# Tail of a two-layer FFN on one core: VectorE's h cos(h) goes to SBUF, GpSimd takes the tail's low parts, and 16 unread products are dropped

## What is computed

```python
h = np.maximum(x @ w_in, 0.0);  x = h * h @ w_out        # layer 1
h = x @ w_in2;  g = h * np.cos(h);  return g @ w_out2    # layer 2
```

## Time and profile before

| what | value |
|---|---|
| median of 3 runs | 1177.63 us |
| the profiled execution, its own time | 1177.56 us |
| its span, first to last instruction | 1175.7 us |
| TensorE busy (matmuls) | 1172.7 us, 100% |
| VectorE, ScalarE, GpSimd busy | 960.4, 806.1, 366.3 us |
| granted TensorE clock, mean | 1.000 |
| the tail, first L1254 to last used product | 1127.1 to 1170.75 us |

### The profile page before, as it was taken

The page is one execution under the profiler, slowest core; times in us unless marked ns, Lnnn a source line. Parts: engine busy times, 40 slices in busy tenths (PEclk is TensorE's granted clock), DMA queues, the critical chain, the costliest instruction groups (busy, mean ns, idle before and its releaser), DMA issues.

```text
span 1175.7 us, 25787 instructions
## 1 busy us (share of the span) xinstructions
PE 1172.7 (100%) x9953; PEld 1132.5 (96%) x9954; DVE 960.4 (82%) x1504; ACT 806.1 (69%) x1467; POOL 366.3 (31%) x265
## 2 busy tenths in 40 slices
PE   9999999999999999999999999999999999999999
PEld 7989999999999999999999999999999999999988
DVE  7968899878878787887878878787787878878787
ACT  4977666667667666666766666676666767666676
POOL 4993634070420706125070430705215070000000
DMA  8511111110111101111011111101111000100001
GB/s 214 135 51 30 35 28 35 17 37 15 23 35 28 35 11 19 35 28 35 15 19 34 25 35 28 35 9 21 35 28 35 13 17 3 26 2 15 1 1 28
DMA packets 113174, 37.33 MB, mean 32 GB/s; under 512 B 101662, under 2 KB 110878, under 8 KB 113052
## 3 DMA queue, kind: packets, MB, share of 16 engines
q1 hardware_dynamic: 111100, 34.87, 14.2%
q10 hardware_dynamic: 1952, 0.80, 0.3%
HBM read 23.84 MB, written 6.29 MB: 26 GB/s over the span
## 4 chain that ended last, share of the span: by engine, by line
PE 100%; issue 0%; DVE 0%
PE y L608 51%; PE h L608 46%; PE y L713 1%; PE h L630 1%; PE h L1121 0%; PE h L637 0%; PE y L674 0%; PE h L640 0%; PE h L644 0%; PE h L1123 0%; PE y L675 0%; PE y L676 0%; PE y L725 0%; DVE g_hi L1543 0%; PE y L659 0%
## 5 line engine op out<-in xcount | busy, mean ns | idle before, releaser
L608 PE MATMUL y<-g_hi,wo 64*128 64x512 f32 x3048 | 698.2, 393 | 0.2
L608 PE MATMUL y<-g_lo,wo 64*128 64x512 f32 x2032 | 521.1, 391 | 0.0
L608 PEld LDWEIGHTS y<-g_hi,wo 64*128 64x128 f32 x3048 | 420.5, 184 | 14.5 <-PE y L608 1.1
L529 POOL TENSOR_TENSOR tap<-xc,gen 128x768 f32<-128x768 f32 x98 | 150.9, 1546 | 575.3 <-DVE xd_lo L1522 555.2
L608 PEld LDWEIGHTS y<-g_lo,wo 64*128 64x128 f32 x2032 | 305.3, 184 | 2.0
L1179 ACT ACTIVATE turns<-turns 128x512 f32<-128x512 f32 x238 | 150.2, 631 | 182.4 <-DVE turns L1473 182.4
L608 PE MATMUL h<-xa_hi,wa_hi 64*128 64x512 f32 x1018 | 270.6, 397 | 0.1
L608 PE MATMUL h<-xa_hi,wa_lo 64*128 64x512 f32 x1018 | 266.0, 391 | 0.0
L608 PE MATMUL h<-xa_lo,wa_hi 64*128 64x512 f32 x1018 | 265.5, 391 | 0.0
L1493 DVE TENSOR_TENSOR h<-h,turns 128x512 f32<-128x512 f32 x238 | 165.6, 696 | 114.6 <-ACT turns L1179 114.2
L1467 DVE SCALAR_TENSOR_TENSOR h<-h,relu 128x512 f32<-128x512 f32 x249 | 173.4, 696 | 57.2 <-ACT relu L1154 55.0
(11 more groups left out here) (127 smaller groups left out, 1092.7 us busy)
## 6 DMA issues: line engine op xcount, KB each, us to landing
xc<-in_x_dram SPq DMA_DIRECT2D x60, 240.0 KB
out_dram<-arena SPq DMA_DIRECT2D x62, 64.0 KB, 1.9
xt_a<-x_blocks SPq DMA_DIRECT2D x224, 16.0 KB, 1.8
arena<-in_moe_w_out_dram SPq DMA_DIRECT2D x16, 192.0 KB, 3.7
arena<-in_moe_w_in_dram SPq DMA_DIRECT2D x16, 128.0 KB, 2.5
out_dram<-arena SPq DMA_DIRECT2D x62, 32.0 KB, 1.7
xt_d<-x_blocks SPq DMA_DIRECT2D x112, 16.0 KB, 1.8
arena<-in_moe_w_in_dram SPq DMA_DIRECT2D x16, 64.0 KB, 2.9
```

Of the source, the lines that this page charges most:

```text
L529: pool.tensor_tensor(tap[:, k % 2, :].rearrange("p (r g) -> p r g", g=GROUP), rows[k], wk, ALU.mult).then_inc(pool_step, 1)
L608: return pe.matmul(o, w[rows, :], x[rows, :], start=start, stop=stop)
```

## The change

In the tail, the product writes 2 pi h cos(h) to SBUF, in `tail_g` (the memory of layer 1's `relu`); the high part is a plain copy of that, and the low part is `tail_g` minus `g2_hi`. The low parts of chunks 238 to 253 are made by GpSimd, those of 254 and 255 by VectorE. TensorE's waits for a free bank go over to the product (`g2_made`), save for the first two such chunks, 240 and 241, whose banks are last read outside the tail's code. VectorE's product waits for the low part of two chunks before, which reads the same half of `tail_g`. The 16 unread products are left out.

```diff
+        tail_g = relu
...
+        POOL_LOWS = range(TAIL - LAG, STEPS - 2)
...
+            for m in POOL_LOWS:
+                pool.wait_ge(g2_hi_ready, m + 1)
+                if m == POOL_LOWS[0]:
+                    pool.wait_ge(g2_ready, m)
+                pool.tensor_tensor(g2_lo[:, m % 2, :], tail_g[:, m % 2, :], g2_hi[:, m % 2, :],
+                                   ALU.subtract).then_inc(g2_ready, 1)
...
-                pe.wait_ge(g2_ready, m - 2)
+                pe.wait_ge(g2_made, m - 2)
...
-                        pe.wait_ge(g2_ready, m - 3)
+                        pe.wait_ge(g2_ready if m - 4 < TAIL - LAG else g2_made, m - 3)
...
-            spare = g2_hi[:, 0, :]
-            line = spare[:, 0:4].unsqueeze(1).to_broadcast([P, TOK // 4, 4])
-            pairs = spare.rearrange("p (b n two) -> p n b two", b=2, two=2)
-            lines = spare.rearrange("p (b n four) -> p n b four", b=2, four=4)
-            for j, moving in enumerate((line, pairs, lines)):
-                for _ in range(4):
-                    pe.matmul(h[:, j, :], wo[1][:, j, 0:P], moving, start=True, stop=True)
-            for _ in range(4):
-                pe.matmul(h[:, 3, :], wo[1][:, 3, 0:DD].bitcast(mybir.dt.bfloat16),
-                          spare[:, 0:TOK // 2].bitcast(mybir.dt.bfloat16), start=True, stop=True)
...
-                        act.activation(g2_hi[:, 1 - c, cols], h[:, tail_bank(m - 1 + part), cols], ACT.Copy,
-                                       scale=2.0 * math.pi).then_inc(g2_hi_ready, 1)
+                        act.activation(g2_hi[:, 1 - c, cols], tail_g[:, 1 - c, cols],
+                                       ACT.Copy).then_inc(g2_hi_ready, 1)
...
-                if m > TAIL - LAG:
+                if m > POOL_LOWS[-1] + 1:
+                    dve.wait_ge(g2_ready, m - 1)
                     for part, cols in parts(m - 1):
                         dve.wait_ge(g2_hi_ready, m + part)
-                        dve.scalar_tensor_tensor(g2_lo[:, 1 - c, cols], h[:, tail_bank(m - 1 + part), cols],
-                                                 2.0 * math.pi, g2_hi[:, 1 - c, cols], ALU.mult,
-                                                 ALU.subtract).then_inc(g2_ready, 1)
+                        dve.tensor_tensor(g2_lo[:, 1 - c, cols], tail_g[:, 1 - c, cols], g2_hi[:, 1 - c, cols],
+                                          ALU.subtract).then_inc(g2_ready, 1)
                 if m < STEPS:
+                    if m >= TAIL - LAG + 2:
+                        dve.wait_ge(g2_ready, m - 1)
                     for part, cols in parts(m):
-                        o = h[:, tail_bank(m + part), cols]
                         dve.wait_ge(cos_ready, m + 1 + part)
-                        dve.tensor_tensor(o, o, wave[:, c, cols], ALU.mult).then_inc(g2_made, 1)
+                        dve.scalar_tensor_tensor(tail_g[:, c, cols], h[:, tail_bank(m + part), cols], 2.0 * math.pi,
+                                                 wave[:, c, cols], ALU.mult, ALU.mult).then_inc(g2_made, 1)
```

## The result

The changed kernel takes 1179.55 us (median of 22 runs, 1179.43 to 1179.70), the kernel before in the same comparison 1177.66 us: 1.89 us more, a ratio of 1.0016 with a 95% interval of 1.0010 to 1.0021. The forecast was 1178.8 us: the side was right, and the cost of the change was put at 1.1 us instead of 1.89.

What follows compares the result with a forecast made beforehand. TensorE was taken to bound the kernel, with VectorE off the path. Gains of 0 and four tail stops totalling 1.14 us on 1177.56 gave 1178.70; the median's 0.07 made it 1178.8 us, range 1177.4 to 1180.8.

Steps and rivals of the forecast that it cites:

- TensorE is the bound, and VectorE's time is off the path: Tail: TensorE sets the pace; 11.0 us less on VectorE only becomes idle time, since products wait for sines: gain 0.
- GpSimd's 1.30 us and the way of 2.05 us: Tail: 1.30 us per GpSimd low part; 2.05 us from high part's start to matmul, 0.60+0.08+1.30+0.07.
- Which chunks: Tail: TensorE stops at chunks 238 (0.55 us), 242 (0.29), 244 (0.16) and 252 (0.14), none at the others.
- steady slots: Tail slots for which chunk 250 stands: low part ready at 1159.68 against matmul at 1159.80, so no stop.
- the forecast's own rule: Tail, per chunk: high part's start plus 2.05 us against the start of the matmul reading the low part; the excess stops TensorE.
- The sum: Whole kernel: stops in the tail total 1.14 us, added to 1177.56 us; with the median's 0.07, 1178.8 us.
- Product and high part in SBUF for nothing: Tail: product written to SBUF, no change; high part read from SBUF, at most 0.02 us a chunk, counted as nothing.
- The end products for nothing: Kernel's end: leaving out the 16 unread products gains 0, as the output does not need them; bounds 0 and 0.9 us.
- The rival that GpSimd paces the tail: Tail: longer GpSimd low parts lose time every two slots; 1181.7 us at 1.85 us each, deciding from 1.65; chance 0.14.
- the margin of 0.12 us: Steady tail slots, read from chunk 250: the low part is ready 0.12 us before its matmul; thin, but no stop.

## Why the prediction was right

*TensorE is the bound, and VectorE's time is off the path: right.* VectorE lost 9.6 us of work and nothing came earlier; its products still start behind sines (12.9 us of waits for L1265).

*GpSimd's 1.30 us and the way of 2.05 us: right.* It measured 1297 ns in the mean. For chunk 238 the high part starts at 1130.16 and the matmul at 1132.22: 2.06 us.

*Which chunks.* 238, 242, 244 and 252 were forecast and are there, in the order of size forecast, and steady slots such as that of 250 have no stop. 248 was not forecast. The run with ScalarE's code moved shows that it is the late issue of its high part: put on time, the stop goes. ScalarE of the kernel before already had that high part 0.66 us behind its L1254, where chunk 249 has 0.51 (its rows, and TensorE's matmul that reads the low part of 248):

```profile
1152.42 0.60 ACT L1254 ACTIVATE turns<-h 128x512 int32<-128x512 f32 x1 [0.44 <-PE h L608]
1153.08 0.60 ACT L1261 ACTIVATE g_hi<-h 128x512 fp32r<-128x512 f32 x1
...
1154.73 0.60 ACT L1254 ACTIVATE turns<-h 128x512 int32<-128x512 f32 x1 [0.32 <-PE h L608]
1155.24 0.60 ACT L1261 ACTIVATE g_hi<-h 128x512 fp32r<-128x512 f32 x1
...
1155.06 0.39 PE L608 MATMUL y<-g_lo,wo 64*128 64x512 f32 x1
```

By the forecast's own rule, 1153.08+2.05 = 1155.13 against 1155.06 is a stop of 0.07. I had read one steady chunk for all. The other 0.17 of its 0.24 us come from the high part, which is later still in the changed kernel (0.84 instead of 0.66).

*The sum: short by 0.75 us.* Forecast were stops of 0.55, 0.29, 0.16 and 0.14; the slots grew by 0.67, 0.43, 0.30 and 0.22, and by 0.34 for chunk 248. The term that was mis-sized is the stop itself: I took it as the lateness of the operand, which was read well (0.55, 0.33, 0.20 and 0.15). With two halves of the array side by side, a stop also costs the new start, 0.10 to 0.12 us in slots 241, 245 and 247 and 0.03 in the last one, 0.35 us in all. The chunk left out is 0.34, and the small rest is lateness a little above the forecast (0.09) and the wait for the high part of 255 (0.04), less 0.06 us in slots 248 to 250.

*Product and high part in SBUF for nothing: off by a size that did not matter much.* In the changed kernel the way from a high part's start to GpSimd's is 0.70 to 0.72 instead of 0.68. With all low parts on VectorE the detour showed 0.3 us.

*The end products for nothing: right,* by two runs.

*The rival that GpSimd paces the tail* was priced by a low part of 1.65 us and more, and did not occur: the 16 low parts took 1289 to 1308 ns, beside a busy VectorE. The run with 0.16 us more on GpSimd cost 0.43 us, and the first steady slots lost 0.04 to 0.11 us, so the margin of 0.12 us was about right.

Still open is what holds an engine for 0.2 to 0.5 us at certain places of its program. On ScalarE the place moved with the code, at unchanged addresses; on VectorE the run that moved the code moved addresses too. The DMA view ties a transfer to these places. It has a queue of kind "instruction", and in the 1 us from the start of the late instruction it shows one transfer of 8192 bytes: in the changed kernel (chunk 248, 1154.80 to 1155.80) and in the one with all low parts on VectorE (chunk 238, 1131.17 to 1132.17). In order:

```profile
q14 instruction: 1, 0.01, 3.3%
...
q14 instruction: 1, 0.01, 3.0%
```

The transfers start 0.65 and 0.67 us after the late instructions. The same stretch has none in the kernels where the code was moved and the instruction is on time. So the late places go with the loading of instructions. Since the transfer seen starts behind the late instruction, it is not what that instruction waited for, and the mechanism is not shown.

Nor was a version tried in which TensorE asks later without waiting for itself.

## What to carry to other kernels

Before work is moved to a slower engine because the faster one is full, look for the matmul that reads its result and subtract: start of the operand's source, plus all durations and handovers, against that matmul's start, chunk by chunk and not in one typical chunk. Neighbouring stops share one lag and must not be added; each one that was left cost a new start on top here. Keep tiles' addresses in mind when two versions are compared: here an added tile was worth more than the change in question.

## What the runs showed of the hardware

The distance of 64 bytes is worth 2.75 us in 1177. The main loop's slots (start of one L1154 to the next, median) are 4.43 us in all kernels without the 64-byte tile ahead of `g2_hi` and 4.41 in those with it. The mean over the loop differs by less, 0.011 us, and over 255 slots that makes the 2.9 us. TensorE in order of time in the kernel before (two products of the two halves together, x2, and how long both are):

```profile
400.32 0.52 PE L608 MATMUL h<-xa_lo,wa_hi 64*128 64x512 f32 x2
400.55 0.52 PE L608 MATMUL h<-xa_hi,wa_lo 64*128 64x512 f32 x2
400.79 0.52 PE L608 MATMUL h<-xd_hi,wd_hi 64*128 64x512 f32 x2
```

and in the kernel before with the 64-byte tile:

```profile
400.00 0.46 PE L609 MATMUL h<-xd_hi,wd_hi 64*128 64x512 f32 x2
400.24 0.46 PE L609 MATMUL h<-xd_hi,wd_lo 64*128 64x512 f32 x2
```

A product takes 0.39 us in both, so the halves run 0.13 us apart in these rows of the first and 0.07 in those of the second. With 128 bytes they are 0.10 apart (0.49) and the time is that of before; so they are in the kernel before without its end products, whose addresses are unchanged. From pair to pair it is 0.23 us in both, so these rows do not show where the slot gets shorter, and whether the distance is a cause is not shown. What in the addresses does this was not found; that it is the addresses was, for the kernels differ in nothing else. The instruction that starts late for no visible reason, and moves when four instructions are put ahead of it, was the other thing not expected: 0.46 us from its operand to VectorE's low part of chunk 238 in two kernels, against 0.10 where it is on time, and 0.66 to 0.86 us from one instruction to the next at ScalarE's high part of chunk 248 in most, against 0.50.
